# The six weight and table loads of a fused attention kernel move to ScalarE's DMA queue

## The reference

```python
for t in range(S):                                   # 1: gated linear attention
    state = alpha[:, :, t, :, None] * state + einsum('bhd,bhe->bhde', k[:, :, t], v[:, :, t])
    y[:, :, t] = einsum('bhd,bhde->bhe', q[:, :, t], state)
gate = sigmoid(causal_conv(x, conv_w))               # 2: five taps, each feature by itself
z = (gate * (x @ w_val)) @ w_out
u = z + real(fft(fft(z, axis=1), axis=2))            # 3: Fourier mixing, then an MLP
out = u + relu(layernorm(u) @ w_ch1) @ w_ch2
```

## Time and profile before

| | |
|---|---|
| median of 3 runs | 588.84 us (588.84 to 588.99) |
| the profiled execution | 591.47 us |
| its span, first to last instruction | 589.7 us |
| TensorE busy | 573.9 us, 97% |
| VectorE busy | 399.8 us, 68% |
| ScalarE busy | 199.1 us, 34% |
| q1, SyncE's queue | 32.32 MB, 16.2% of the 16 engines |
| mean granted clock of TensorE | 0.993 |

### The profile page before, as it was taken

The page is one execution under the profiler, slowest core; times in us unless marked ns, Lnnn a source line. Parts: engine busy times, 40 slices in busy tenths (PEclk is TensorE's granted clock), DMA queues, the critical chain, the costliest instruction groups (busy, mean ns, idle before and its releaser), DMA issues.

```text
span 589.7 us, 12408 instructions
## 1 busy us (share of the span) xinstructions
PE 573.9 (97%) x5173; PEld 544.0 (92%) x5173; DVE 399.8 (68%) x891; ACT 199.1 (34%) x441; POOL 14.0 (2%) x31
## 2 busy tenths in 40 slices
PE   7999999999999999999999999999999999999996
PEld 6788999999999999999999999999999999999995
DVE  7579989978948676886948476877855574542221
ACT  4333355424333144324133133322433223322220
POOL 0000000000000000000000000000000000000000
PEclk7999999999999999999999999999999999999999
DMA  7658001232222002043202002022100000000000
GB/s 273 220 160 372 1 19 53 70 113 73 71 79 71 27 1 70 20 122 97 70 5 93 28 2 70 2 92 94 53 1 28 1 27 2 1 1 28 10 18 27
DMA packets 16858, 37.84 MB, mean 64 GB/s; under 512 B 2337, under 2 KB 5410, under 8 KB 16546
## 3 DMA queue, kind: packets, MB, share of 16 engines
q1 hardware_dynamic: 14976, 32.32, 16.2%
q0 software_dynamic: 1536, 4.72, 2.2%
q10 hardware_dynamic: 290, 0.01, 0.0%
HBM read 32.32 MB, written 4.72 MB: 63 GB/s over the span
## 4 chain that ended last, share of the span: by engine, by line
PE 91%; DVE 5%; issue 2%; ACT 1%; DMA 0%; POOL 0%; DVEq 0%
PE bank L897 44%; PE bank L982 24%; PE evens L929 4%; PE sums L938 3%; PE bank L1008 2%; PE evens L954 2%; PE evens L962 2%; PE evens L967 2%; PE bank L1079 2%; PE sums L924 1%; PE bank L1045 1%; PE bank L1089 1%; PE bank L1014 1%; DVE unT_lo L648 1%; PE evens L957 1%
## 5 line engine op out<-in xcount | busy, mean ns | idle before, releaser
L879 DVE SCALAR_TENSOR_TENSOR h_lo<-bank,h_hi 128x256 fp32r<-128x256 f32 x144 | 60.6, 422 | 100.7 <-ACT h_hi L641 98.0
L897 PE MATMUL bank<-unT_hi,w_hi 128*128 128x256 f32 x432 | 125.4, 290 | 2.7 <-DVE unT_lo L648 2.2
L897 PE MATMUL bank<-unT_lo,w_hi 128*128 128x256 f32 x432 | 122.1, 283 | 0.0
L897 PE MATMUL bank<-unT_hi,w_lo 128*128 128x256 f32 x432 | 121.6, 282 | 0.0
L641 ACT ACTIVATE h_hi<-bank 128x256 fp32r<-128x256 f32 x144 | 54.9, 381 | 174.0 <-PE bank L897 174.0
L982 PE MATMUL bank<-w_hi,h_hi 128*128 128x384 f32 x288 | 99.3, 345 | 0.0
L982 PE MATMUL bank<-w_lo,h_hi 128*128 128x384 f32 x288 | 97.6, 339 | 0.0
L982 PE MATMUL bank<-w_hi,h_lo 128*128 128x384 f32 x288 | 97.2, 338 | 0.0
L897 PEld LDWEIGHTS bank<-unT_hi,w_hi 128*128 128x128 f32 x432 | 81.2, 188 | 9.3 <-DVE unT_lo L648 4.9
L897 PEld LDWEIGHTS bank<-unT_hi,w_lo 128*128 128x128 f32 x432 | 81.6, 189 | 0.0
L897 PEld LDWEIGHTS bank<-unT_lo,w_hi 128*128 128x128 f32 x432 | 81.4, 189 | 0.0
(11 more groups left out here) (186 smaller groups left out, 1078.6 us busy)
## 6 DMA issues: line engine op xcount, KB each, us to landing
a_in<-in_alpha_dram SPq DMA_DIRECT2D x24, 258.5 KB, 2.7
q_in<-in_q_dram SPq DMA_DIRECT2D x24, 256.0 KB, 2.7
k_in<-in_k_dram SPq DMA_DIRECT2D x24, 256.0 KB, 3.1
v_in<-in_v_dram SPq DMA_DIRECT2D x24, 224.0 KB, 3.3
w_raw<-in_w_dram SPq DMA_DIRECT2D x2, 2304.0 KB, 11.6
out_dram<-u POOLq DMA_DIRECT2D x24, 192.0 KB, 2.3
dftd<-in_dft_d_dram SPq DMA_DIRECT2D x1, 582.0 KB, 6.4
woutT<-in_w_out_t_dram SPq DMA_DIRECT2D x1, 576.0 KB, 7.2
```

The costliest lines, as they stand in the source:

```text
L879: dve.scalar_tensor_tensor(h_lo[:, f % HBUF, :], ps[:, 0:GW], 0.0, h_hi[:, f % HBUF, :].bitcast(F32), ALU.max, ALU.subtract).then_inc(s_re ...
L897: last = pe.matmul(ps, l, r, start=(i == 0), stop=(i == len(mms) - 1))
```

## The change

SyncE now issues only the chunks' loads. ScalarE issues dft, woutT, wval, wout, cos and nsin directly behind its three small loads, with no wait and ahead of its first computation; it issues w1 behind the copy of the first `wd` (a == 0) and w2 behind that of the third (a == K - 1). SyncE's wait for the last `wd` goes. Sizes, buffers, semaphores of the loads and the schedule stay.

```diff
-            srcs = {"wval": w_val, "wout": w_out, "w1": w1, "w2": w2, "cos": fold_cos, "nsin": fold_nsin}
-            beside = {1: ("fourier",), 2: ("wval",), 3: ("wout",), 4: ("cos", "nsin"), 5: ("w1", "w2")}
-
             for b in range(B):
                 for c in range(NCH):
                     load_chunk(b, c)
-                    for name in beside.get(c, ()) if b == 0 else ():
-                        if name == "fourier":
-                            sp.dma_start(dftd[:, :, :], dft_d).then_inc(s_dload, 16)
-                            sp.dma_start(woutT[:, :, :], w_out_t).then_inc(s_dload, 16)
-                        else:
-                            if name == "w2":
-                                sp.wait_ge(s_unit, done(("wd", 0, K - 1, 0)))
-                            sp.dma_start(w_raw[name][:, :, :], srcs[name]).then_inc(s_wload[WN.index(name)], 16)
...
             act.dma_start(oddr_raw[:, :], odd_row).then_inc(s_small, 16)
+
+            def load_weight(name, src):
+                act.dma_start(w_raw[name][:, :, :], src).then_inc(s_wload[WN.index(name)], 16)
+
+            act.dma_start(dftd[:, :, :], dft_d).then_inc(s_dload, 16)
+            act.dma_start(woutT[:, :, :], w_out_t).then_inc(s_dload, 16)
+            load_weight("wval", w_val)
+            load_weight("wout", w_out)
+            load_weight("cos", fold_cos)
+            load_weight("nsin", fold_nsin)
...
                     act.activation(wd_hi[:, a, :], ps[:, 0:2 * NC], ACT.Copy).then_inc(s_hi, 1)
+                    if a == 0:
+                        load_weight("w1", w1)
+                    elif a == K - 1:
+                        load_weight("w2", w2)
```

## The result

The changed kernel is slower: 593.94 us median (593.58 to 595.16, 4 runs) against 588.91 (588.84 to 588.99, 4 runs) for the kernel before. The ratio is 1.0089, 95% interval 1.0072 to 1.0107, so about +5.0 us, where +2.6 (591.4) was forecast and the range ended at 592.5. The profiled execution took 594.05 us with a span of 592.3. That span is just what the prediction gave for it, and that is the first clue: against its own profiled partner, 591.47 us and 589.7, the changed kernel lost 2.6 us; against the timed runs it lost 5.0.

A forecast was written before the change was run, and what follows sets the result against it. TensorE, busy 97% of the span, was taken as the bound. Delays of 1.6 us at `sums` and 0.5 at `y`, plus the late clock, made +2.6 on 588.84, so 591.4 us; range 589.4 to 592.5.

The forecast's parts named there:

- the delay lies inside the span and is added to each alike: Final step: the same delay added to the 588.84 us timed median and the 591.47 us profiled execution, giving 591.4 and 594.1.
- 1.6 us of `sums`: Chunk 0 on TensorE: `sums` waits for the late kdT and starts at 12.5, 1.6 us late (bounds 1.1 and 2.4).
- 0.5 of `y`: Chunk 0 on TensorE: late masks of chunk 1 hold `y` to 15.0 instead of 14.5; 0.5 us (bounds 0, and rival 2).
- 0.5 of clock: TensorE's clock rises late, a third of `wd` 0 at the low level, taking the delay from +2.1 to +2.6 us.
- The cover of 0.73 us: Chunk 0: 0.73 us of scores matmuls (10.20 to 10.93) hide part of kdT's delay before `sums` waits.
- The issue term: Six issues hold ScalarE 3.1 us (bounds 2.6 and 3.9); after 0.74 us of idle time, kdT is 2.3 us late.
- a full queue: Stated way to be wrong: an issue on ScalarE takes much more than 0.6 us because the queue is full.
- The shares of 31%: Early DMA: engines alternate 2 KB chunk packets with 4.5 KB dft packets, so chunk loads get 31% of the bandwidth.
- chunk loads land past 13: Stated sign that the prediction is wrong: loads of chunks landing later than 13 us.
- the forecast's own 17 for k of chunk 1: k of chunk 1 lands near 17 us, when all is through; counted as no cost.
- Rival 2: Chunk loads get far less than 31%: 596 if the new queue goes first, 592.2 half-way; chance 0.11.
- No matmul waits for a weight: TensorE in the unchanged kernel: no matmul waits for a weight or later chunk, so a freer queue removes no wait.

The follow-up runs named there:

- the run with fillers: Changed kernel with 17 warm-up matmuls instead of 12 and 14 unused identity matmuls between scores and `sums` of chunk 0; 592.01 us median.
- diag late: Changed kernel with the diag step moved behind the scores of chunk 0, the six issues and their traffic kept; 593.91 us median.
- the traffic run: Changed kernel with the diag step behind the scores of chunk 0 and 22 warm-up matmuls instead of 12; 591.28 us median.
- Small loads: Kernel before plus six 7.5 KB loads issued by ScalarE: 593.21 us; with 17 warm-ups and 12 unused matmuls ahead of `sums`, 590.98 us.
- the GpSimd run: Changed kernel with the six first weight and table loads issued by GpSimd, w1 and w2 still by ScalarE; 591.44 us median.
- the other: Second profiled execution of the kernel before, no edit, chunk 0 at 2.4 GHz throughout; 589.35 us, span 587.6.

## Why the prediction was wrong

*Direction and chain.* Right: slower, by ScalarE's issues ahead of kdT, `sums` waiting for kdT, no gain from a freer queue, w1 and w2 free.

*The step that failed: "the delay lies inside the span and is added to each alike".* The profiled execution took 591.47 us, all timed runs 588.84 to 588.99. I noted both times, left the 2.6 us between them unexplained, and added the delay of the one to the other. The gap was the clock: in the profile chunk 0 ran at 1.2 GHz, in the timed runs at 2.4. Between two executions that both lose the clock the change costs what I forecast (594.05 - 591.47 = 2.6), but in part by luck. I had added 1.6 us of `sums`, 0.5 of `y` and 0.5 of clock; in the two profiles `sums` starts 2.8 us later (13.70 against 10.93), and neither `y` nor `wd` 0 adds to that. The timed runs had the clock to lose, and lost it: 1.9 us by the run with fillers, on top of the delay. Forecast and rivals all asked when a clock already low would rise, none whether it was low at all.

*The cover of 0.73 us* belonged to the slow scores of that profile. With the clock high TensorE already waits for kdT, 0.8 us in the kernel before with 17 warm-ups, so the delay of kdT counts in full: 3 us where I had 1.6.

*The issue term was mis-sized:* 3.1 us, measured 4.2 in the profile, 4.0 in the run with fillers and in that with diag late, and 3.6 in the traffic run; my upper bound was 3.9. Small loads take 2.88 and 3.08. Most of the excess is at the fifth issue (0.92 to 1.45 us for cos) and some at the fourth and sixth; the prediction had named a full queue as a way to fail, and that the queue was full is not shown. kdT came 3.35 us late in the profile and 3.05 with the fillers, not 2.3.

*The traffic.* The shares of 31% gave k at 8.1 and the decays of chunk 1 at 12.4. Measured: decays at 10.84, 11.36, 11.66 and 12.31 in four executions, k not late at all in the profile of the changed kernel, and at 7.20, 7.49 and 8.14 in the three others. The estimate lies at the late end of what happens, between no delay and starving. That the sizes of the packets set the shares is not shown by this: the shares would be the same in all four. The sign "chunk loads land past 13" did appear, beside the forecast's own 17 for k of chunk 1: that k landed at 15.1 and the decays of chunk 2 at 18.4, which VectorE waited 0.6 us for. I counted the traffic as 0.5 us beside ScalarE's delay; in the changed kernel it is wholly covered by the later kdT, alone it costs 1.9 to 2.9. Rival 2, starving, did not occur at chunk 1; what came nearest is the 14.2 us of chunk 3's decays in the GpSimd run.

*The terms together*, for the timed runs: delay of kdT 2.9 to 3.05, traffic 0 beside it, clock 1.9, together 4.8 to 5.0; measured 5.0. The issues of small loads alone give 1.9 to 2.0 of the delay; the remaining 1.0 comes with the large loads, whose issues take longer. Whether it is their own size or the busy engines that holds the issue was not separated.

*"No matmul waits for a weight"* was also true only of that profile: in the other, `wd` 0 waits 0.3 us for woutT.

## What to carry to other kernels

Where a profiled execution is off the timed runs by more than their spread, find out why before anything is added to it; here 2.6 us, as much as the whole forecast, sat in that gap. A DMA issue held ScalarE for 0.3 to 1.5 us in order, so on an engine whose first results others wait for it belongs behind those results. A pause of TensorE of 3 to 4 us was paid twice here, in waiting and in the clock afterwards, and matmuls whose results nobody uses, put into the pause, took the second payment away.

## What was not expected of the hardware

The same kernel ends in four narrow groups, 588.8 to 589.4, 590.3 to 590.8, 591.1 to 591.4 and 592.0 to 592.4 us, and the mean granted clock of a run tells its group; five more matmuls at the start left only the first in ten runs. The recorded clock can also miss it: with five warm-up matmuls a run of 591.31 us reads 0.999. Loads beside a queue with larger pieces can take 9.7 us to land instead of 4.4, and 14.2 with a third queue at work.
